# Spreading the rows of later blocks over eleven steps, and routing in seven groups instead of six

## The chip, the cores and the metric

The kernel is one program on one core of a Trainium2 chip. The metric is the device time of one launch in microseconds (us); less is better. The engines are named as the profile names them: PE is TensorE (PEld its weight loads), DVE VectorE, ACT ScalarE, POOL GpSimd, SP SyncE.

## What is computed

Pooled attention, then a sparse layer with 8 experts of which each row takes 2, then a dense layer with 4 experts that all rows take. There are N = 2304 rows of D = 512. Cut to what matters:

```python
x = attention(q, k, v)                       # 18 tiles of 128 rows
noisy = x @ w_gate + log1p(exp(x @ w_noise)) * noise
top2, weights = best two experts of each row, softmax of their noisy logits
for e in range(8):                           # first layer: each row by its two experts
    out[mask] += w * (relu(x[mask] @ w1[e]) @ w2[e])
p = domain_probs / sum(domain_probs)
for e in range(4):                           # second layer: all rows by all four experts
    out2 += p[:, e] * (relu(out @ w1b[e]) @ w2b[e])
```

## The kernel before

Everything is ordered by hand: each engine has its own list of instructions and waits on semaphores; nothing is scheduled for it. Products in float32 are made as three matmuls of a high part and a low part (`PASSES`), so each operand is needed twice: ACT makes the high part, DVE or POOL the low one.

**Attention and routing (0 to 150 us).** One turn of a loop for each of the 18 tiles. `GROUPS` says after which tiles the routing of a group is done: ACT `softplus(g)` one turn after its last tile, DVE `select(g)` two turns after, PE `ranks(g)`, DVE `places(g)` and `pair_weights(g)` three turns after. With the places known, POOL's `scatter(g)` issues two indirect DMAs for each tile into `x_sorted`. Only when all 36 have landed does ACT load the first sorted rows.

**First layer (150 to 660 us).** 44 tiles at most, of which the last ones may be empty; an empty tile is skipped by a branch on each engine (`guarded`). ACT stores each tile with `y_store`. Behind it POOL waits for all stores and then gathers.

**Second layer (660 us to the end).** The 2304 rows are three blocks of 768 (blocks 0, 1, 2), the weights 16 units (`UNITS`: 4 experts in 4 quarters), visited twice. Steps 0 to 15 (`SOLO`) are block 0 with units 0 to 15. Steps 16 to 47 are blocks 1 and 2 with each unit in turn (`double`). A step is one `up` (a Strassen-like product of 7 parts, 42 matmuls, with sums on DVE, `hidden`) and one `down` (36 matmuls in six outputs, `accumulate` on DVE). PE's order is up(s), down(s-1), up(s+1), down(s), and so on. The output banks are a ring of three, so output t waits until DVE has added output t-3.

Around the steps there are two other jobs:

- The operands of a block are made from nine pairs of rows tiles. `fetch(n)` on POOL gathers the two expert results of rows tile n (two indirect DMAs), `scale_first(n)` on ACT and `combine(n)` on DVE add them with their weights, `x2_turn(n)` on PE transposes them, and `pair_hi`, `sums_hi` (ACT), `pair_sums`, `pair_lo` (DVE) make the operands of pair i = tiles 2i and 2i+1. Pairs 0 to 2 are block 0, 3 to 5 block 1, 6 to 8 block 2. Block 1's operands are first read in step 16. Pair 6 and later overwrite those of block 0.
- The weights of unit n: SP loads them, POOL makes `weight_sums`, ACT `w1_high(n)` and `w2_high`, POOL `w1_low` and `w2_low`. `up` of the unit waits for `w1_ok`, `down` for `w2_ok`.

Before, pairs 3, 4 and 5 are made in steps 1 to 3, and rows tiles 12 to 16 in a bunch before steps 14 and 15. POOL starts the weight sums of unit n only when PE has finished the last `up` that reads the buffer (`pool.wait_ge(up_ps, used)`). In each step DVE first finishes the hidden block, with its last two low parts, and then adds the six outputs.

## Time and profile before

| | |
|---|---|
| three runs | 1496.77 us median (1495.77 to 1503.64) |
| the profiled execution | 1504.66 us, of which its span is 1502.6 us |
| PE busy | 1373.0 us (91%) |
| DVE busy | 717.5 us (48%) |
| POOL busy | 647.4 us (43%) |
| ACT busy | 398.0 us (26%) |
| chain that ended last | PE 45%, DVE 3%, issue 2%, POOL, ACT and DMA 1% each |

The profile is of one execution, so times inside it are compared with its own 1504.66 us, not with the median. Its page lists a slot as busy when a matmul is under way, whatever the clock; the granted clock is listed beside it.

### The profile page before, as it was taken

Reading aid. Unit: us, or ns where it says so; the run is one execution under the profiler, and the core shown is the slowest. Engines: PE = TensorE matmul, PEld = TensorE weight load, DVE = VectorE, ACT = ScalarE, POOL = GpSimd, SP = SyncE. Lnnn points to the kernel's source line nnn. Section 1 sums busy time; section 2 is a strip of 40 time slices with the busy share of each in tenths; the row PEclk is TensorE's granted clock in tenths of the full one; section 3 lists DMA queues with packets and bytes.
Section 4 is the critical chain, followed back from the end, with each engine's and each line's share of the span. In section 5 each row is a group of like instructions: output and inputs, shape, how many; then the busy total and the mean of one; then the engine's idle time right before and its main releaser. Section 6 shows DMA issues by size and latency. Waiting matters only on the chain.

```text
span 1502.6 us, 22621 instructions
## 1 busy us (share of the span) xinstructions
PE 1373.0 (91%) x6969; PEld 1206.9 (80%) x6970; DVE 717.5 (48%) x1287; ACT 398.0 (26%) x734; POOL 647.4 (43%) x421
## 2 busy tenths in 40 slices
PE   6884799999999999954589999889999999999999
PEld 5884688888888888844469999779898989989897
DVE  5657422222222222215466666676666565665655
ACT  2443122222222222213233333332222222222311
POOL 1226357275382662724446667633332234222320
PEclk9887799999999999976789999999999999999999
DMA  9737233242332422222212213220010000100002
GB/s 272 254 108 277 73 127 115 82 154 84 112 130 74 151 98 98 85 86 77 72 55 70 70 56 113 92 90 28 29 56 28 28 28 28 55 28 28 14 0 84
DMA packets 64105, 131.86 MB, mean 88 GB/s; under 512 B 4984, under 2 KB 22520, under 8 KB 63992
## 3 DMA queue, kind: packets, MB, share of 16 engines
q1 hardware_dynamic: 45432, 86.79, 17.1%
q0 software_dynamic: 6528, 22.42, 4.8%
q10 hardware_dynamic: 12096, 22.03, 4.3%
q8 instruction: 27, 0.44, 0.1%
q14 instruction: 22, 0.18, 0.0%
HBM read 106.57 MB, written 28.84 MB: 90 GB/s over the span
## 4 chain that ended last, share of the span: by engine, by line
PE 45%; DVE 3%; issue 2%; POOL 1%; ACT 1%; DMA 1%; DVEq 0%; POOLq 0%; ACTq 0%
PE banks L851 24%; PE banks L824 21%; DMA acc<-y_sorted,y_pos_int 1%; POOL unit_w_ops L487 1%; DVE hD L1580 1%; DVE acc L1618 0%; POOL acc L526 0%; DVE x_ops L1576 0%; DVE acc L1551 0%; DVE x_sums L1562 0%; ACT block_sums L1123 0%; ACT hD L1129 0%; DVE x_sums L1565 0%; DVE x_sums L1563 0%; ACT acc L1095 0%
## 5 line engine op out<-in xcount | busy, mean ns | idle before, releaser
L851 PE MATMUL banks<-unit_w,hD 128*128 128x512 f32 x1728 | 405.8, 392 | 7.9 <-DVE acc L1618 6.2
L824 PE MATMUL banks<-x_ops,unit_w_ops 128*128 128x384 f32 x2016 | 368.4, 340 | 37.8 <-ACT block_sums L1123 29.0
L824 PEld LDWEIGHTS banks<-x_ops,unit_w_ops 128*128 128x128 f32 x2016 | 359.5, 192 | 43.9 <-ACT block_sums L1123 30.3
L851 PEld LDWEIGHTS banks<-unit_w,hD 128*128 128x128 f32 x1728 | 322.5, 188 | 78.5 <-DVE acc L1618 10.1
L1618 DVE SCALAR_TENSOR_TENSOR acc<-banks,prob_norm,acc 128x512 f32<-128x512 f32 x270 | 199.0, 747 | 95.0 <-PE banks L851 91.7
L748 PE MATMUL banks<-expert_w,xT 128*128 (+1 forms) x960 | 234.1, 400 | 1.6 <-DVE xT L1405 1.6
L774 PE MATMUL banks<-expert_w,hT 128*128 (+1 forms) x960 | 226.0, 391 | 2.8 <-issue 2.8
L774 PEld LDWEIGHTS banks<-expert_w,hT 128*128 128x128 f32 x960 | 181.3, 189 | 40.7 <-issue 3.0
L748 PEld LDWEIGHTS banks<-expert_w,xT 128*128 128x128 f32 x960 | 180.7, 192 | 39.5 <-issue 1.9
L1518 DVE COPY y_rows<-banks 128x512 f32<-128x512 f32 x40 | 27.6, 691 | 338.9 <-PE banks L774 338.9
L544 POOL TENSOR_TENSOR expert_w<-raw_weights,zeros 128x2048 f32 x28 | 100.8, 3600 | 191.6 <-PE banks L774 173.6
L469 POOL TENSOR_TENSOR weight_sums<-raw_weights 128x256 f32<-128x256 f32 x32 | 24.1, 753 | 356.2 <-PE banks L824 308.7
L547 POOL TENSOR_TENSOR expert_w<-raw_weights,expert_w 128x2048 f32 x28 | 129.1, 4611 | 5.2 <-POOL expert_w L544 5.2
L1580 DVE SCALAR_TENSOR_TENSOR hD<-block_sums,hD 128x384 fp32r<-128x384 f32 x144 | 102.6, 739 | 34.3 <-ACT hD L1125 27.8
L1042 ACT CAST hT<-banks 128x512 fp32r<-128x512 f32 x80 | 43.0, 590 | 205.3 <-PE banks L757 205.3
L487 POOL TENSOR_TENSOR unit_w_ops<-raw_weights,unit_w_ops 128x512 fp32r<-128x512 f32 x64 | 63.7, 1017 | 65.2 <-ACT unit_w_ops L1139 65.1
L1033 ACT ACTIVATE h_rows<-banks 128x512 f32<-128x512 f32 x80 | 43.5, 596 | 181.0 <-PE banks L748 181.0
L491 POOL TENSOR_TENSOR unit_w<-raw_weights,unit_w 128x1024 fp32r<-128x1024 f32 x32 | 76.9, 2402 | 31.8 <-ACT unit_w L1144 31.6
L487 POOL TENSOR_TENSOR unit_w_ops<-weight_sums,unit_w_ops 128x1024 fp32r<-128x1024 f32 x32 | 76.8, 2400 | 0.0
L1507 DVE TENSOR_TENSOR hT<-banks,hT 128x512 fp32r<-128x512 f32 x80 | 51.5, 686 | 50.1 <-ACT hT L1042 50.1
L1123 ACT COPY block_sums<-banks 128x384 f32<-128x384 f32 x48 | 23.0, 480 | 176.2 <-PE banks L824 169.6
L1125 ACT ACTIVATE hD<-block_sums 128x384 fp32r<-128x384 f32 x48 | 25.3, 526 | 152.9 <-DVE block_sums L1597 152.9
(177 smaller groups left out, 1202.7 us busy)
## 6 DMA issues: line engine op xcount, KB each, us to landing
raw_weights<-in_w SPq DMA_DIRECT2D x32, 1024.0 KB
raw_weights<-in_w1b SPq DMA_DIRECT2D x32, 512.0 KB, 3.4
raw_weights<-in_w2b SPq DMA_DIRECT2D x32, 512.0 KB, 3.2
x_rows<-x_sorted ACTq DMA_DIRECT2D x44, 256.0 KB, 2.6
y_sorted<-y_rows ACTq DMA_DIRECT2D x40, 256.0 KB, 2.0
out<-acc SPq DMA_DIRECT2D x18, 256.0 KB, 2.0
qT<-in_q SPq DMA_DIRECT2D x3, 1152.0 KB, 16.5
kv_half<-in_k SPq DMA_DIRECT2D x5, 576.0 KB, 11.6
```

The costliest lines, as they stand in the source:

```text
L487: ins = pool.tensor_tensor(lo, src, hi.bitcast(F32), ALU.subtract)
L491: pool.tensor_tensor(w2o[:, par, 1, :], raw[:, par, 1024:2048], w2o[:, par, 0, :].bitcast(F32), ALU.subtract).then_inc(w2_ok, 1)
L544: pool.tensor_tensor(hi, src, zeros[:, 0:1].to_broadcast([P, 2048]), ALU.add).then_inc(split_no, 1)
L547: pool.tensor_tensor(lo, src, hi.bitcast(F32), ALU.subtract).then_inc(raw_used[r % 2], 1)
L748: mm = pe.matmul(bank[n][:, :], xT[:, u % 2, st, c, :], wall[:, bass.ds(slot, 1), 0, mv, FF * c + 512 * n:FF * c + 512 * n + 512], start=( ...
L774: mm = pe.matmul(bank[5 + u % 2][:, :], hT[:, u % 2, st, c, :], wall[:, bass.ds(slot, 1), 1, mv, D * c:D * c + D], start=(t == 0), stop=(t ...
L824: mm = pe.matmul(dst[:, 0:HALF], w1o[:, par, st, b, c, :], x2o[:, blk, a, mv, c, :], start=(first and t == 0), stop=(t == 5), skip_group_c ...
L851: mm = pe.matmul(bank[5 + t % 3][:, :], hD[:, buf, st, c, P * t:P * t + P], w2o[:, par, mv, D * c:D * c + D], start=(n == 0), stop=(n == 3 ...
L1033: r = act.activation(h_sb[:, 512 * n:512 * n + 512], bank[n][:, :], ACT.Relu)
L1507: d = dve.tensor_tensor(hT[:, u % 2, 1, 4 * n:4 * n + 4, :], bank[2 + n][:, :].rearrange("p (c r) -> p c r", c=4), hT[:, u % 2, 0, 4 * n:4 ...
L1580: dve.scalar_tensor_tensor(out=hD[:, buf, 1, m, at:at + HALF], in0=src, scalar=0.0, in1=hD[:, buf, 0, m, at:at + HALF].bitcast(F32), op0=A ...
L1618: dve.scalar_tensor_tensor(out=to, in0=bank[5 + t % 3][:, :], scalar=p, in1=to, op0=ALU.mult, op1=ALU.add).then_inc(acc_ok, 1)
```

## The change

`GROUPS` gets seven entries instead of six, so that the third group is three tiles and ends one turn earlier. The rest moves work in the second layer:

- DVE: `hidden(s)` takes the outputs of step s-1 with it. Output 0 is added before the last two low parts, outputs 1 to 5 behind them. Extra work (a combine, or a part of a pair) stands behind a given output of a given step; the tables say which. Pairs 3, 4, 5 now come in steps 2, 4, 7, rows tiles 6 to 16 in steps 1, 3, 5, 6, 9, 10, 11.
- POOL: the weight sums no longer wait for PE; ACT's `w1_high` waits in their place.
- POOL no longer looks in the table of tiles which stores to wait for; ACT signals for the empty tiles in a branch.
- The operands of a pair are made in smaller pieces with a signal each, and `up(0)` starts with the products that need only the plain parts.

```diff
-GROUPS = ((0, 4), (4, 8), (8, 12), (12, 15), (15, 17), (17, 18))
+GROUPS = ((0, 4), (4, 8), (8, 11), (11, 13), (13, 15), (15, 17), (17, 18))
...
-            tail = [load_code(pool, j) for j in range(SURE_TILES, TILES_B)]
-            pool.wait_ge(y_out[0], 16 * SURE_TILES // 2)
-            pool.wait_ge(y_out[1], 16 * SURE_TILES // 2)
-            for j in range(SURE_TILES, TILES_B):
-                with pool.If(tail[j - SURE_TILES] // 16 % 2 > 0):
-                    pool.wait_ge(y_out[j % 2], 16 * (j // 2 + 1))
+            for i in range(2):
+                pool.wait_ge(y_out[i], 16 * TILES_B // 2)
...
+            for n in range(2, SOLO + 2):
+                if n == 2:
+                    pool.wait_ge(x2T_ps, BT)
+                    for r in range(BT, BT + 3):
+                        fetch(r)
+                w1_sums(n, n % 2, n // 2 + 1)
...
+                w1_lows(n, n % 2)
+                if n == 3:
+                    pool.wait_ge(x2_ok, BT + 2)
+                    fetch(BT + 3)
...
+                if n > 2:
+                    w2_of(n - 1, (n - 1) % 2)
+                if n == 9:
+                    pool.wait_ge(x2T_ps, 2 * BT)
+                    for r in range(2 * BT, 2 * BT + 3):
+                        fetch(r)
...
-            up(0, 0, 0)
+            product(0, 0, A11, B11, bank[0]).then_inc(up_ps, 1)
+            product(0, 0, A22, T4, bank[4])
+            pe.wait_ge(m1_ok, 1)
+            product(0, 0, A12, B21, bank[0], first=False)
+            pe.wait_ge(x2_sum_hi, 6)
             pairs_read(3)
+            product(0, 0, S2, T2, bank[1]).then_inc(up_ps, 1)
+            product(0, 0, S3, T3, bank[2]).then_inc(up_ps, 1)
+            product(0, 0, S1, T1, bank[3]).then_inc(up_ps, 2)
+            pe.wait_ge(cx, 3)
+            product(0, 0, S4, B22, bank[3], first=False).then_inc(up_ps, 1)
+
+            turns = {2: 3, 4: 4, 7: 5}
+            for n in range(1, 8):
                 pe.wait_ge(w1_ok, n + 1)
-                pairs_read(n + 1 if n > 1 else 3)
+                if n - 1 in turns:
+                    pairs_read(turns[n - 1] + 1)
                 up(n, n % 2, 0)
-                pair_turn(n + 2)
+                if n in turns:
+                    pair_turn(turns[n])
                 pe.wait_ge(w2_ok, n)
                 down(n - 1, (n - 1) % 2, (n - 1) % 2)
...
+                with act.If(codes[u] // 16 % 2 > 0):
+                    y_store(g, u)
+                with act.Else():
+
+                    act.wait_ge(y_out[u % 2], 16 * (j // 2))
+                    act.sem_inc(y_out[u % 2], 16)
...
+            scaled = {1: (6, 7), 3: (8, 9), 5: (10,), 6: (11,), 9: (12, 13), 10: (14, 15), 11: (16,), 15: (17,)}
+            turned = {2: 3, 4: 4, 7: 5, 15: 6, 16: 8}
+            for s in range(SOLO):
+                h_hi_d(s, s % 2)
+                if s in turned:
+                    pair_hi(turned[s])
+                    sums_hi(turned[s])
+                for n in scaled.get(s, ()):
+                    scale_first(n)
+                w1_high(s + 2, s % 2, 6 * s + 6)
+                if s:
+                    w2_high((s + 1) % 2, (s + 1) // 2 + 1, BT * s)
...
+                if outputs:
+                    outputs(0)
                 dve.wait_ge(hD_hi, 4 * s + 3)
                 low(buf, 0, HALF, three)
                 dve.wait_ge(hD_hi, 4 * s + 4)
                 low(buf, 1, 0, both)
+                if outputs:
+                    for t in range(1, BT):
+                        outputs(t)
...
+            extras = {1: rows_in(6, 7), 2: pair_in(3), 3: rows_in(8, 9), 4: pair_in(4), 5: rows_in(10), 6: rows_in(11),
+                      7: pair_in(5), 9: rows_in(12, 13), 10: rows_in(14, 15), 11: rows_in(16)}
```

**How the order moves.** First ACT, from the end of the hidden block of step 0 to the start of that of step 1. In the rows `acc<-acc,pair_weights` is `scale_first`, `unit_w_ops` are the three casts of `w1_high(2)`, and `block_sums<-banks` is the copy in `h_hi_d(1)` on whose signal PE waits in `up(1)`. Before:

```order
L1129 ACTIVATE hD<-block_sums 128x384
L1131 ACTIVATE hD<-block_sums 128x384
L1095 ACTIVATE acc<-acc,pair_weights 128x512 x3
L1137 CAST unit_w_ops<-raw_weights 128x512
L1138 CAST unit_w_ops<-raw_weights 128x256
L1139 CAST unit_w_ops<-weight_sums 128x1024
L1095 ACTIVATE acc<-acc,pair_weights 128x512
L1123 COPY block_sums<-banks 128x384
```

And after the change:

```order
L1141 ACTIVATE hD<-block_sums 128x384
L1143 ACTIVATE hD<-block_sums 128x384
L1151 CAST unit_w_ops<-raw_weights 128x512
L1152 CAST unit_w_ops<-raw_weights 128x256
L1153 CAST unit_w_ops<-weight_sums 128x1024
L1135 COPY block_sums<-banks 128x384
```

The four `scale_first` (rows tiles 6 to 9) no longer stand ahead of the copy; the three casts still do.

Then DVE in step 1: `block_sums` and `hD` are the hidden block, `acc<-banks,prob_norm` an output of step 0, `acc<-acc,pair_weights` a `combine`, `x_sums` and `x_ops` a pair. Before:

```order
L1591 TENSOR_TENSOR block_sums<-banks,block_sums 128x384
L1594 TENSOR_TENSOR block_sums<-banks,block_sums 128x384
L1597 TENSOR_TENSOR block_sums<-banks,block_sums 128x384
L1580 SCALAR_TENSOR_TENSOR hD<-block_sums,hD 128x384
L1580 SCALAR_TENSOR_TENSOR hD<-banks,hD 128x384
L1603 TENSOR_TENSOR block_sums<-block_sums,banks 128x384
L1605 TENSOR_TENSOR block_sums<-block_sums,banks 128x384
L1580 SCALAR_TENSOR_TENSOR hD<-block_sums,hD 128x384 x2
L1551 SCALAR_TENSOR_TENSOR acc<-acc,pair_weights 128x512
L1562 TENSOR_TENSOR x_sums<-banks,x_sums 128x256
L1563 TENSOR_TENSOR x_sums<-banks,x_sums 128x256
```

And after the change:

```order
L1576 TENSOR_TENSOR block_sums<-banks,block_sums 128x384
L1559 SCALAR_TENSOR_TENSOR hD<-block_sums,hD 128x384
L1559 SCALAR_TENSOR_TENSOR hD<-banks,hD 128x384
L1582 TENSOR_TENSOR block_sums<-block_sums,banks 128x384
L1584 TENSOR_TENSOR block_sums<-block_sums,banks 128x384
L1605 TENSOR_SCALAR acc<-banks,prob_norm 128x512
L1559 SCALAR_TENSOR_TENSOR hD<-block_sums,hD 128x384 x2
L1605 TENSOR_SCALAR acc<-banks,prob_norm 128x512
L1523 SCALAR_TENSOR_TENSOR acc<-acc,pair_weights 128x512
L1605 TENSOR_SCALAR acc<-banks,prob_norm 128x512
L1523 SCALAR_TENSOR_TENSOR acc<-acc,pair_weights 128x512
L1605 TENSOR_SCALAR acc<-banks,prob_norm 128x512 x3
```

The pair has left the step, the first output stands ahead of the last two low parts, and the two combines stand between later outputs.

## Rows read from the trace of the kernel before

**Rows 1.** Windows: stretch, length, busy PE, PEld, DVE, ACT, POOL, PEclk, DMA share, GB/s

```profile
705.00:790.00 85.00, 55.99 (x259) 48.59 (x260) 45.63 (x73) 26.98 (x48) 39.69 (x35) 0.84 0.16 56
...
922.00:1010.00 88.00, 77.67 (x372) 67.18 (x372) 61.99 (x96) 31.96 (x56) 49.26 (x42) 0.96 0.28 93
...
1010.00:1503.00 493.00, 489.38 (x2455) 442.35 (x2453) 299.92 (x472) 117.73 (x212) 143.84 (x113) 1.00 0.10 34
```

**Rows 2.** Waits of TensorE: engine, line, releaser, total us, times, longest

```profile
PE banks L824 <- ACT block_sums L1123: 29.0, 4, 13.0
...
PE banks L729 <- DMA x_rows<-x_sorted: 17.5, 1, 17.5
```

**Rows 3.** Timeline, TensorE, first steps of the second layer (start, us, what, idle before)

```profile
704.99 4.40 PE L824 MATMUL banks<-x_ops,unit_w_ops 128*128 128x384 f32 x24 [1.26 <-DVE block_sums L1605]
...
722.38 6.13 PE L824 MATMUL banks<-x_ops,unit_w_ops 128*128 128x384 f32 x18 [12.98 <-ACT block_sums L1123]
...
771.73 7.47 PE L824 MATMUL banks<-x_ops,unit_w_ops 128*128 128x384 f32 x42
...
789.96 7.47 PE L824 MATMUL banks<-x_ops,unit_w_ops 128*128 128x384 f32 x42
```

**Rows 4.** The chain that ended last, one undisturbed step (start, us, what)

```profile
821.23 7.30 PE banks L824 x42
828.53 8.23 PE banks L851 x36
```

**Rows 5.** Timeline, ScalarE, just before TensorE's wait at 722 us ends

```profile
721.24 0.72 ACT L1095 ACTIVATE acc<-acc,pair_weights 128x512 f32<-128x512 f32 x1 [12.01 <-DMA acc<-y_sorted,y_pos_int]
```

**Rows 6.** Timeline, GpSimd, the weight sums of one unit: first and last

```profile
703.87 0.73 POOL L469 TENSOR_TENSOR weight_sums<-raw_weights 128x256 f32<-128x256 f32 x1 [6.08 <-issue]
...
706.38 0.93 POOL L474 TENSOR_TENSOR weight_sums<-weight_sums,raw_weights 128x256 f32<-128x256 f32 x1
```

**Rows 7.** Timeline, TensorE, the steps around the change of blocks

```profile
929.83 7.47 PE L824 MATMUL banks<-x_ops,unit_w_ops 128*128 128x384 f32 x42
...
989.36 4.43 PE L824 MATMUL banks<-x_ops,unit_w_ops 128*128 128x384 f32 x24
...
1009.84 7.47 PE L824 MATMUL banks<-x_ops,unit_w_ops 128*128 128x384 f32 x42
```

**Rows 8.** Timeline, GpSimd's scatters, and the first gather behind them

```profile
129.80 0.96 POOL L453 DMA_INDIRECT x_sorted<-x_sb,pos_int  x1 [1.66 <-DVE pos_int L1366]
...
146.05 1.14 POOL L453 DMA_INDIRECT x_sorted<-x_sb,pos_int  x1 [0.30 <-issue]
...
151.87 0.39 ACTq L1017 DMA_DIRECT2D x_rows<-x_sorted  x1
```

**Rows 9.** Timeline, last store and first fetch; from the page, a store's landing

```profile
661.16 0.36 ACTq L1049 DMA_DIRECT2D y_sorted<-y_rows  x1
...
665.36 0.99 POOL L526 DMA_INDIRECT acc<-y_sorted,y_pos_int  x1 [34.43 <-issue]
...
y_sorted<-y_rows ACTq DMA_DIRECT2D x40, 256.0 KB, 2.0
```

**Rows 10.** Timeline, block 0: last transpose, last low parts (DVE), first product

```profile
688.49 1.11 PE L810 MATMUL banks<-ident,acc 128*128 128x128 f32 x4 [1.61 <-DVE acc L1551]
...
693.25 1.22 DVE L1576 TENSOR_TENSOR x_ops<-x_sums,x_ops 128x1024 fp32r<-128x1024 f32 x1 [0.18 <-ACT x_ops L1113]
...
694.74 8.99 PE L824 MATMUL banks<-x_ops,unit_w_ops 128*128 128x384 f32 x42 [5.14 <-DVE x_ops L1576]
```

**Rows 11.** Timeline, VectorE's low part of a hidden block, alone and beside GpSimd

```profile
857.76 0.56 DVE L1580 SCALAR_TENSOR_TENSOR hD<-block_sums,hD 128x384 fp32r<-128x384 f32 x1 [0.59 <-ACT hD L1125]
...
935.23 2.41 POOL L491 TENSOR_TENSOR unit_w<-raw_weights,unit_w 128x1024 fp32r<-128x1024 f32 x1
...
935.45 2.60 DVE L1580 SCALAR_TENSOR_TENSOR hD<-block_sums,hD 128x384 fp32r<-128x384 f32 x1 [0.59 <-ACT hD L1125]
```

**Rows 12.** Timeline, ScalarE, a late start in the attention stage

```profile
99.71 0.79 ACT L935 COPY expT<-banks 96x768 f32<-96x768 f32 x1 [5.50 <-remote]
```

254 lines of the change are left out of this document (86 added, 168 removed).

## The prediction

> **What bounds the kernel now.** I read the windows first. From 1010 us to the end PE is busy without a gap at full clock; it is not in the 85 us from 705, where the clock is 0.84 and PE is busy for 56.0, nor in the 88 us from 922, where it is busy for 77.7 [rows 1]. The chain of waits confirms that full stretches are PE's own time: one undisturbed step is 7.30 us of `up` and 8.23 us of `down`, 15.53 in all, with nobody else in it [rows 4]. So only what refills PE in the disturbed stretches can give time.
>
> The waits by releaser name two large ones: 29.0 us in four waits for the copy of the block sums on ACT, and 17.5 us in one wait for the first sorted rows [rows 2]. The timeline shows the longest of the four: 24 matmuls of `up(1)` from 704.99, then 12.98 us of nothing, then 18 matmuls that take 6.13 us [rows 3]. At the full clock 18 of 42 are 18/42 x 7.30 = 3.13 us, so the wait also costs 3.0 us of clock. The copy is short, but on ACT it stands behind a `scale_first` that began only at 721.24, after 12.01 us in which ACT had nothing to do but wait for its rows to land [rows 5]. The bound there is the order on ACT, not its load.
>
> **The change, term by term** (against the profiled execution's 1504.66 us).
>
> *Routing, -2.7.* Before, twelve scatters run from 129.80 to 146.05, the last start: (146.05 - 129.80)/11 = 1.48 us each, and the gather of rows is issued 151.87 - 146.05 = 5.8 us behind the last start [rows 8]. These twelve are tiles 12 to 17. With the new groups tile 12 goes with (11, 13), whose places come two turns earlier, in time that POOL has free; ten scatters stay behind the places of (13, 15), which come in the same turn as before. That is two scatters less: 2 x 1.48 = 3.0. The seventh group costs DVE, PE and ACT some small instructions in the turns before, so I take -2.7; its bounds are -1.4 (one scatter) and -4.5 (three). Behind it stands the 17.5 us wait, so it shortens one to one.
>
> *End of the first layer, +2.* The last store is issued at 661.16 and lands 2.0 us later; the first fetch is issued at 665.36 [rows 9]. Of the 2.2 us between, some 0.3 is the start, as between two scatters, so POOL's last branch in and its four for the empty tiles take 1.9, about 0.4 each. They go, but ACT must now walk through its own before it gives the last signal: behind the store 12 guarded pieces and two loads of the table. No row times one of these; at POOL's 0.4 each, 661.52 + 14 x 0.4 = 667.1, and the fetch 0.3 behind, 2 us later than now. Lower bound: they hide behind the landing, and POOL's saved branches give 1 us. Upper bound: ACT's are half as dear again, +5. I take +2, by the nearest row.
>
> Advanced Engine Details and Errata of the Trainium skill (Control Flow Timing) gives about 108 ns for a compare-and-branch and 51 ns for a jump; by that the term would be about zero. No row here shows it.
>
> *Operands of block 0 and up(0), -2.6.* The last transpose starts at 688.49, the first product at 694.74, right behind the low parts of the sums; these start at 693.25 for 1.22 us, after DVE had stood 0.18 [rows 10]. The plain low parts were ready at 693.07. The new order starts with products that need only these: 694.74 - 693.07 = 1.7 less. The signals are finer too: the first sum starts a transpose early, and casts and low parts of the sums overlap by halves. I put that at about 0.6 in each of the three rounds, an estimate from pieces of 0.3 to 0.6 us (bounds 0 and 1): 1.7 + 1.7 = 3.4. Inside `up(0)` the last product now waits for a DVE sum (0.56 for such a size [rows 11], and the way there and back) that the two plain products used to cover: +0.8.
>
> *First refill, -30.* From the start of `up(1)`, 704.99, to that of `up(4)`, 789.96, are 84.97 us [rows 3] for three steps. The step with pair 5, 771.73 to 789.96, is 18.23 [rows 3], so a pair costs 18.23 - 15.53 = 2.7: eight transposes and the outputs that DVE adds late. New: three steps and one pair, 3 x 15.53 + 2.7 = 49.3. Two pairs are paid later: + 5.4. 84.97 - 49.3 - 5.4 = 30.3.
>
> This needs that nothing new is late at `up(1)`. ACT: the hidden block of step 0, then the three casts of `w1_high(2)` (about 2 us), then the copy. PE runs 24 matmuls, 4.40 us, before it needs the copy, and 1.26 us pass before it starts [rows 3]. ACT ends the hidden block about 2 us behind `up(0)` (four short pieces, DVE sums of 0.56 between them): 2 + 2 + 0.5 = 4.5 against 5.66. POOL: the weight sums that the casts wait for take 706.38 + 0.93 - 703.87 = 3.4 us [rows 6] behind six fetches of about 1.3 us, together 11.3 from the last transpose, while `up(0)` alone ends some 12.5 from there. No wait, with 1.2 us to spare on each side. Rows tiles 6 and 7 have one step more to land, tile 9 two.
>
> *Change of blocks, -10.5.* From 929.83 to 1009.84 [rows 7] are 80.0 us for four ups and four downs. New: 4 x 15.53 = 62.1, two pairs 5.4, two more transposes 0.8, and about 1.2 for the last product of `up(16)` behind the sums: 69.5. The rows are combined in steps 9 to 11; a late tile can't hold the copy, and output 0 is added before the low parts, so a held-up low part no longer holds PE. `up(16)` keeps its place, 989.36, relative to pair 6: pair 7 can't be made before the banks of the outputs are free.
>
> *A pair in its new place, +1.* The low parts of a pair now stand behind output 2, not 0, and the next `up` waits for them: by my count of DVE's work they end 8.5 us into a `down` of 8.2 to 9. Five pairs, 0.2 each; bounds 0 and +5.
>
> *Everything else, 0.* The weight sums start earlier in each step, beside other work of DVE; PE needs the weights a step later. Output 0 lands about 2.2 us into a `down`, and the ring needs it at 4.1.
>
> Sum: -2.7 + 2 - 2.6 - 30.3 - 10.5 + 1 = -43. On the profiled execution 1504.66 - 43 = 1461.6. That execution was 7.9 above the median; the trace doesn't show where, and I take none of it as removed. So on the median 1496.77 - 43 = **1454**.
>
> **Rivals.**
>
> *A wait takes the place of the first (12 in 100).* The margins at `up(1)` are about 1 us. If the fetches are slow, ACT stands before the weight sums instead of before the rows, and PE's clock falls again. The waits at the change of blocks still go. The worst likely is one wait of half the old size with its clock, 12.98/2 + 3 = 9.5, and as much in a later step: about -43 + 19 = -24, **1473**. For it: POOL's queue is serial, and ACT's too. Against: nothing lands late in the count above.
>
> *Instruction supply (8 in 100).* The loops of ACT, DVE and POOL over steps 4 to 13 become straight code. ACT starts a copy at 99.71 after 5.50 us idle that no wait explains [rows 12], in straight code while the DMA queues are full. Two such gaps, with little hidden by slack, add 4 to 8: **1458 to 1462**. Runtime: NRT & Kernel Launch of the Trainium skill (Instruction fetch mechanics) says that straight code is fetched ahead and a taken branch out of the window is what stalls; by that rule this change gains at the loops and the new branches of ACT lose. The trace shows only the gap, not its cause.
>
> *Slower (4 in 100): DVE and POOL hold each other in every step.* A low part of the hidden block takes 0.56 us alone and 2.60 while POOL's subtraction runs [rows 11]. The weight sums now start beside this low part, in 46 steps. Followed through the step, output 0 would be ready at about 2.9 instead of 2.2 us; the ring asks for it at 4.1, so a hold of 2.04 costs nothing. It costs from about 2.9 us of hold on, and to eat 43 us and end **above 1504** it must be 2.9 + 50/46 = 4.0 us in each step. Two of POOL's 2.41 us instructions in a row would do it. GPSIMD Engine Reference of the Trainium skill (1. Specifications) says that the two share SBUF interfaces when a DVE instruction has two SBUF inputs, as this one has; the row agrees, and the rule speaks against moving the sums.
>
> *No effect (4 in 100).* The stretches are as long as before, because the rows, not ACT's order, set them: **1490 to 1500**. Against: ACT waits for rows of block 1, which no product reads before step 16.
>
> **How the numbers follow.** Forecast 72 in 100, its own range 1446 to 1463 from the bounds: routing +1.3 and -1.8, stores -3 and +3, pairs -1 and +4, change of blocks +3 and -2. The range to state reaches to the first rival, 1445 to 1470. About 0.5% (7.5 us) is what a measurement of this kernel tells from no change. Faster 0.92, same 0.04, slower 0.04.
>
> **What would show it.** Right: no wait over 2 us for the copy of the block sums, full clock from the second product of the layer on, steps of 15.5 us with 18 in steps 2, 4 and 7; the first gather about 149; the first fetch 6 us behind the last store. Wrong: ACT waiting for weight sums or rows inside steps 1 to 3, low parts of a pair ahead of an `up` that waits, low parts of 3 us and more in each step beside POOL, or idle without a releaser in the straight code.

## The result and the profile after

The changed kernel takes 1458.05 us (median of 4 runs, 1455.32 to 1460.38); the kernel before took 1496.27 us beside it (4 runs). The ratio is 0.974, with a 95% interval of 0.9694 to 0.9785: faster. The forecast was 1454 us, range 1445 to 1470.

The profiled execution of the changed kernel took 1460.38 us (its span is 1458.7 us), which is 44.3 us less than the 1504.66 us of the profiled execution before. The forecast by terms, made for that pair, was -43, or 1461.6 us. The medians differ by 38.2 us only; the interval of the ratio allows 32 to 46 us, and the experiments show what scatters (below).

The page of the changed kernel, its busy PE and the granted clock in 40 slices:

```profile
PE 1361.3 (93%) x6970; PEld 1197.4 (82%) x6971; DVE 706.5 (48%) x1310; ACT 396.8 (27%) x746; POOL 638.0 (44%) x421
PE   6885699999999999992999999999999999999999
PEclk9977799999999999995999999999999999999999
```

One weak slice is left at the border of the two layers. The timeline of TensorE there, for the changed kernel (start us, us, what, and in brackets the idle time before and who ended it):

```profile
690.03 8.57 PE L818 MATMUL banks<-x_ops,unit_w_ops 128*128 128x384 f32 x36 [2.89 <-issue]
699.25 1.32 PE L818 MATMUL banks<-x_ops,unit_w_ops 128*128 128x384 f32 x6 [0.65 <-DVE block_sums L1576]
701.84 7.54 PE L818 MATMUL banks<-x_ops,unit_w_ops 128*128 128x384 f32 x42 [1.26 <-DVE block_sums L1584]
...
717.42 7.47 PE L818 MATMUL banks<-x_ops,unit_w_ops 128*128 128x384 f32 x42
724.73 1.04 PE L804 MATMUL banks<-ident,acc 128*128 128x128 f32 x8
725.52 8.75 PE L845 MATMUL banks<-unit_w,hD 128*128 128x512 f32 x36
735.14 7.55 PE L818 MATMUL banks<-x_ops,unit_w_ops 128*128 128x384 f32 x42 [0.88 <-issue]
...
750.73 7.47 PE L818 MATMUL banks<-x_ops,unit_w_ops 128*128 128x384 f32 x42
```

Against [rows 3]: the wait inside `up(1)` and the slow 18 matmuls behind it are gone, and from the start of `up(1)` to that of `up(4)` are 750.73 - 701.84 = 48.89 us, not 84.97. The one pair in these three steps, turned at 724.73, costs a `down` of 8.75 us and 0.88 us of wait ahead of the next `up`.

The windows of the changed kernel, the first steps of the second layer and the long last stretch (columns as in [rows 1]):

```profile
701.84:787.00 85.16, 83.40 (x424) 74.57 (x424) 61.86 (x99) 36.52 (x65) 60.02 (x49) 1.00 0.23 78
965.30:1458.70 493.40, 489.33 (x2455) 442.46 (x2454) 289.10 (x474) 116.15 (x212) 133.28 (x109) 1.00 0.10 35
```

In the same length in which PE was busy for 56.0 us at a clock of 0.84 [rows 1] it is busy for 83.4 at full clock.

At the change of blocks the kernel before lost the most in `up(15)`, again by a row that ScalarE scales ahead of the copy. These are its TensorE and its ScalarE there:

```profile
972.54 5.79 PE L824 MATMUL banks<-x_ops,unit_w_ops 128*128 128x384 f32 x18 [3.88 <-ACT block_sums L1123]
```

```profile
970.46 0.72 ACT L1095 ACTIVATE acc<-acc,pair_weights 128x512 f32<-128x512 f32 x1 [9.73 <-DMA acc<-y_sorted,y_pos_int]
```

In the changed kernel nothing waits for the copy there. Inside `up(16)` a wait of 2.25 us is left, and the timeline shows where it is from, first on TensorE, then on VectorE:

```profile
944.40 6.50 PE L818 MATMUL banks<-x_ops,unit_w_ops 128*128 128x384 f32 x36
953.15 1.62 PE L818 MATMUL banks<-x_ops,unit_w_ops 128*128 128x384 f32 x6 [2.25 <-DVE block_sums L1576]
```

```profile
947.95 2.21 DVE L1552 TENSOR_TENSOR x_ops<-x_sums,x_ops 128x512 fp32r<-128x512 f32 x1
950.08 1.22 DVE L1555 TENSOR_TENSOR x_ops<-x_sums,x_ops 128x512 fp32r<-128x512 f32 x1
951.22 0.55 DVE L1570 TENSOR_TENSOR block_sums<-banks,block_sums 128x384 f32<-128x384 f32 x1
951.87 0.56 DVE L1573 TENSOR_TENSOR block_sums<-banks,block_sums 128x384 f32<-128x384 f32 x1
952.53 0.56 DVE L1576 TENSOR_TENSOR block_sums<-banks,block_sums 128x384 f32<-128x384 f32 x1
```

Pair 7's low parts (L1552, L1555) take 2.21 and 1.22 us there beside GpSimd, where pair 6's took 0.68 each, and three block sums stand behind them; the last product of `up(16)` needs the third of these.

Last, the end of the first layer in the changed kernel, the last store on ScalarE's queue and the first fetch on GpSimd:

```profile
658.46 0.35 ACTq L1057 DMA_DIRECT2D y_sorted<-y_rows  x1
```

```profile
663.99 0.99 POOL L526 DMA_INDIRECT acc<-y_sorted,y_pos_int  x1 [35.64 <-ACTq L1084]
```

5.53 us lie between them, against 4.20 in [rows 9]; GpSimd is released by L1084, the signal in ScalarE's `Else`.

### The profile page after: what moved, and what is told of

The parts are those of the page before. It is cut to its first block, busy times and chain, and to the rows that moved or that the text cites. A ratio compares the mean times of both kernels' runs of the same rounds, so it can differ in the third digit from the quotient of the medians.

```text
span 1458.7 us, 22255 instructions
## 1 busy us (share of the span) xinstructions
PE 1361.3 (93%) x6970; PEld 1197.4 (82%) x6971; DVE 706.5 (48%) x1310; ACT 396.8 (27%) x746; POOL 638.0 (44%) x421
## 4 chain that ended last, share of the span: by engine, by line
PE 51%; DVE 2%; issue 1%; DMA 0%; ACT 0%; POOL 0%; DVEq 0%; POOLq 0%
PE banks L845 26%; PE banks L818 24%; PE banks L804 1%; DVE acc L1602 0%; DVE x_ops L1555 0%; DVE acc L1523 0%; DMA acc<-y_sorted,y_pos_int 0%; POOL acc L526 0%; DVE hD L1559 0%; DVE x_ops L1552 0%; DVE x_sums L1536 0%; DVE x_ops L1544 0%; DVE x_ops L1546 0%; ACT x_ops L1118 0%; DVE x_sums L1538 0%
## 5 line engine op out<-in xcount | busy, mean ns | idle before, releaser
L818 PE MATMUL banks<-x_ops,unit_w_ops 128*128 128x384 f32 x2016 | 361.8, 337 | 10.0 <-issue 4.7
L818 PEld LDWEIGHTS banks<-x_ops,unit_w_ops 128*128 128x128 f32 x2016 | 353.6, 189 | 15.9 <-issue 9.0
L487 POOL TENSOR_TENSOR unit_w_ops<-raw_weights,unit_w_ops 128x512 fp32r<-128x512 f32 x64 | 67.7, 1078 | 363.8 <-ACT unit_w_ops L1153 363.7
L1559 DVE SCALAR_TENSOR_TENSOR hD<-block_sums,hD 128x384 fp32r<-128x384 f32 x144 | 87.7, 637 | 28.6 <-ACT hD L1137 28.4
L453 POOL DMA_INDIRECT x_sorted<-x_sb,pos_int x36 | 37.1, 1031 | 55.6 <-DVE pos_int L1338 46.2
```

The lines of the kernel that those rows point to most:

```text
L487: ins = pool.tensor_tensor(lo, src, hi.bitcast(F32), ALU.subtract)
L818: mm = pe.matmul(dst[:, 0:HALF], w1o[:, par, st, b, c, :], x2o[:, blk, a, mv, c, :], start=(first and t == 0), stop=(t == 5), skip_group_c ...
L1559: dve.scalar_tensor_tensor(out=hD[:, buf, 1, m, at:at + HALF], in0=src, scalar=0.0, in1=hD[:, buf, 0, m, at:at + HALF].bitcast(F32), op0=A ...
```

## A ruler for the experiments

The whole times were taken in three groups, by the record on three chips: b_again, before_order, sums_wait and out0_last on chip 4; before_orders, bunched2, pool_asks and six_groups on chip 6; banks_only, up0_old, best1 and best2 on chip 14. The kernel before took 1497.02, 1487.96 and 1497.16 us beside them. So whole times compare across groups only as ratios to the kernel before, and the absolute times that some expectations name are some 9 us too high for the second group.

Single terms are smaller than what whole runs scatter, so each is read between two landmarks inside the trace. They are: the last product of the routing's gate on TensorE; the first gather; the last store of the first layer; the first fetch; the starts of `up(0)`, `up(1)`, `up(8)`, `up(15)`, `up(17)`; the end. In us, from the starts of the rows (the first five columns are lengths):

| kernel | gate to gather | store to fetch | fetch to up(1) | up(1) to up(8) | up(17) to end | gate at | gate to end |
|---|---|---|---|---|---|---|---|
| before | 20.28 | 4.20 | 39.63 | 147.14 | 492.8 | 131.59 | 1371.0 |
| before, again | 20.34 | 4.19 | 39.81 | 146.73 | 492.8 | 131.50 | 1368.1 |
| changed | 18.42 | 5.53 | 37.85 | 115.77 | 493.4 | 131.87 | 1326.8 |
| before_order | 20.08 | 4.20 | 41.28 | 138.19 | 492.9 | 126.01 | 1363.7 |
| before_orders | 20.88 | 4.20 | 39.71 | 122.11 | 492.5 | 110.92 | 1346.2 |
| sums_wait | 18.57 | 5.53 | 38.76 | 117.36 | 493.4 | 129.84 | 1332.7 |
| out0_last | 18.40 | 5.54 | 37.96 | 113.49 | 492.2 | 131.63 | 1322.9 |
| bunched2 | 18.79 | 5.54 | 37.86 | 117.03 | 493.4 | 119.74 | 1326.6 |
| pool_asks | 18.48 | 4.19 | 38.50 | 117.35 | 493.4 | 113.49 | 1327.9 |
| six_groups | 20.92 | 5.56 | 37.97 | 115.77 | 493.4 | 114.72 | 1329.5 |
| banks_only | 18.67 | 5.54 | 38.63 | 113.75 | 493.4 | 139.88 | 1327.2 |
| up0_old | 18.50 | 5.54 | 37.41 | 115.76 | 494.5 | 128.44 | 1327.4 |
| best1 | 18.59 | 4.18 | 38.57 | 112.77 | 492.2 | 135.95 | 1320.0 |
| best2 | 13.81 | 4.18 | 37.16 | 111.21 | 492.3 | 134.07 | 1312.5 |

The column "gate at" is the stage that no experiment touches but for its groups, and it spreads over 29 us: 110.92 to 119.74 us on chip 6, 126.01 to 139.88 us in all others. "Gate to end" leaves it out. Where `up(1)` itself takes 9.1 us in place of 7.5 (sums_wait, pool_asks, banks_only, best1), the clock is at its full level later; below this is called the late clock. The windows from 701 to 709 us of the changed kernel and of sums_wait, both around `up(1)`:

```profile
701.00:709.00 8.00, 7.16 (x41) 7.19 (x42) 4.97 (x9) 4.15 (x8) 4.72 (x4) 1.00 0.00 0
```

```profile
701.00:709.00 8.00, 6.93 (x31) 6.96 (x32) 4.34 (x8) 3.53 (x7) 5.94 (x7) 0.79 0.00 0
```

Nearly the same busy time holds 41 matmuls at a clock of 1.00 and 31 at 0.79. That is worth some 2.2 us over `up(0)` and `up(1)` (pool_asks against the changed kernel). No edit is common to the four kernels that have it, and pool_asks changes nothing there; what decides it was not tested.

## The experiments

### The kernel before, once more

> The kernel before, unchanged, profiled once more: to see which stretches vary from one execution to the next. Its profiled execution took 1504.66 us where the median of its runs is about 1496. If the surplus of 8 us sat in the first refill, the second trace shows less than 84.97 us from the start of up(1) to that of up(4), and the forecast gain there was too large by as much. If it sat in the routing stage (TensorE's waits for ScalarE's transposes and VectorE's keys), the refill is again 84 to 86 us and the stretch up to the first gather (151.87 us) is shorter by some microseconds. If the long last stage held it, the 492.76 us from up(17) to the end shrink.

It took 1501.71 us. The refill is as long as in the first trace: from `up(1)`, 702.22, to `up(4)`, 786.81, are 84.59 us. The gate stands at 131.50. The 3.0 us that this execution is shorter lie in the first layer, between the first gather and the last store. So the two executions differ outside the part that the change touches. Where the other 5 of the 8 us over the median lie is open, since this execution is above its median too.

### Only row 9, only on ScalarE (in the kernel before)

```diff
             w1_high(2, 0)
-            scale_first(BT + 3)
             h_hi_d(1, 1)
+            scale_first(BT + 3)
             pair_copy(3)
```

> The kernel before with one line moved: ScalarE scales row 9 behind its four copies of the hidden values of step 1 and no longer ahead of them. Theory (ScalarE's order held the copies behind a row that had not landed): the wait of 12.98 us inside up(1) [rows 3] is gone, and with it part of the low clock behind it: 10 to 16 us faster than before, about 1481 to 1486 us; the waits for rows 10 and 11 stay or shrink. Rival one (GpSimd's weight sums, which waited for the products of the step before, set the pace of the refill): no more than 3 us gained, the wait moves to the weights. Rival two (rows simply land too late for whoever needs them): the time of the wait comes back at the turn of pair 4, less than 5 us gained.

1489.5 us where before took 1497.02, ratio 0.9939 (0.9915 to 0.9964): 7.5 us in the median, and 8.5 us between `up(1)` and `up(4)`, 76.09 where the second trace of before has 84.59. That is less than the 10 to 16 expected of the theory and more than either rival gave. The timeline of TensorE in this kernel says why:

```profile
705.50 3.41 PE L824 MATMUL banks<-x_ops,unit_w_ops 128*128 128x384 f32 x18 [0.23 <-ACT block_sums L1123]
...
720.61 7.00 PE L851 MATMUL banks<-unit_w,hD 128*128 128x512 f32 x18 [6.74 <-DVE acc L1621]
...
742.68 5.17 PE L824 MATMUL banks<-x_ops,unit_w_ops 128*128 128x384 f32 x18 [10.88 <-ACT block_sums L1123]
```

and of its ScalarE and VectorE:

```profile
716.51 0.72 ACT L1095 ACTIVATE acc<-acc,pair_weights 128x512 f32<-128x512 f32 x1 [4.66 <-DMA acc<-y_sorted,y_pos_int]
717.14 0.35 ACT L1102 COPY x_sums<-banks 128x256 f32<-128x256 f32 x1
...
741.54 0.72 ACT L1095 ACTIVATE acc<-acc,pair_weights 128x512 f32<-128x512 f32 x1 [7.63 <-DMA acc<-y_sorted,y_pos_int]
```

```profile
717.35 0.75 DVE L1551 SCALAR_TENSOR_TENSOR acc<-acc,pair_weights 128x512 f32<-128x512 f32 x1 [3.77 <-ACT acc L1095]
```

The 12.98 us wait is 0.23 now. But VectorE also works in order: it combines row 9 at 717.35, makes the sums of pair 3 and adds the outputs of `down(0)` only behind that, so `down(0)` stands 6.74 us for a free bank. Those sums need copies of the pair as well, and on ScalarE these still stand behind row 9 (717.14). So the row holds VectorE twice, by its own combine and by ScalarE's copies of the pair; no run parts the two. And `up(2)` still waits for the copy that stands behind row 11. Half of the first stall came back one product later.

### Three rows on ScalarE, two of them on VectorE (in the kernel before)

```diff
@@ ScalarE
-            scale_first(BT + 3)
             h_hi_d(1, 1)
             ...
             w1_high(3, 1)
-            scale_first(BT + 4)
+            scale_first(BT + 3)
             w2_high(0, 2, BT)
-            scale_first(BT + 5)
             h_hi_d(2, 0)
+            scale_first(BT + 4)
             ...
             w1_high(4, 0)
+            scale_first(BT + 5)
@@ VectorE
             hidden(1, 1)
-            combine(BT + 3)
             pair_in(3, 0, 0)
-            combine(BT + 4)
+            combine(BT + 3)
             hidden(2, 0)
+            combine(BT + 4)
             pair_in(4, 1, 1)
```

(Row 11 keeps its place on VectorE, behind pair 4.)

> The kernel before with rows 9, 10 and 11 taken in later on both engines that work in order: ScalarE scales row 9 behind the hidden copies of step 1 and the pair turned there, row 10 behind the copies of step 2, row 11 behind that step's pair; VectorE combines each of them behind the outputs that stood behind it. GpSimd's late weight sums, the steps in which pairs are turned and everything else stay as before. From the kernel with row 9 moved on ScalarE alone, which went from up(1) to up(4) in 76.1 us (84.6 in the kernel before again) with a wait of 6.74 us for VectorE behind row 9 and one of 10.88 us behind row 11. Theory (the place of the rows in the order of both engines is the cause): both are gone and up(1) to up(4) takes 53 to 60 us, the whole 1468 to 1476 us. Rival (a row needs three pairs in three steps too soon, so that the changed kernel's spread over eight steps is what pays): the waits come back at the turns of pairs 4 and 5, up(1) to up(4) takes 68 us or more, the whole over 1482 us.

1462.68 us where before took 1487.96 beside it, ratio 0.9843 (0.981 to 0.9875). From `up(1)` to `up(4)` are 684.12 to 744.05, 59.9 us, at the upper end of the theory's 53 to 60; up to `up(8)` it is 122.11 us. In medians it is 25 us faster than before, so order alone brings 25 of the changed kernel's 31 us there (147.14 - 122.11 of 147.14 - 115.77). No wait of over 2.3 us is left in the first steps:

```profile
699.00 1.66 PE L851 MATMUL banks<-unit_w,hD 128*128 128x512 f32 x6 [1.84 <-DVE acc L1621]
701.72 3.02 PE L851 MATMUL banks<-unit_w,hD 128*128 128x512 f32 x12 [1.06 <-DVE acc L1621]
...
721.50 4.49 PE L851 MATMUL banks<-unit_w,hD 128*128 128x512 f32 x12 [2.24 <-DVE acc L1618]
```

These are outputs 1 and 2 of a `down`, late behind the pair's sums on VectorE, since output 0 and the pair stand there in one block. The changed kernel puts each part of a pair behind an output of its own, which fits the other 6 us; no run isolates it.

### GpSimd's weight sums wait again (in the changed kernel)

```diff
-            def w1_sums(n, par, turn):
+            def w1_sums(n, par, turn, used):
                 pool.wait_ge(w1_in[par], 16 * turn)
+                pool.wait_ge(up_ps, used)
```

> The changed kernel with GpSimd's weight sums of a step waiting again until the products of the step two before have been taken in, as in the kernel before. Theory (the order on ScalarE was the cause, the earlier sums are worth little): 0 to 3 us slower than the changed kernel, that is 1458 to 1461 us, the loss at the first one or two steps, where the weights come about 3.4 us behind up(0). Rival (the earlier sums are what freed the refill): 13 us or more slower, and TensorE waits for the weights' last operands at every step from up(1) on.

1462.76 us, ratio 0.9762 (0.972 to 0.9803), just above the theory's 1458 to 1461. From `up(2)` to `up(8)` it takes 819.43 - 719.20 = 100.2 us, in the changed kernel 817.61 - 717.42 = 100.2: nothing. `up(1)` is 1.6 us longer, by its clock (above), and from `up(15)` to `up(17)` 2.0 us are lost, 41.05 against 39.03. The rival's 13 us are not there. The earlier sums are worth about 2 us, at the change of blocks.

### Output 0 last (in the changed kernel)

```diff
                 dve.tensor_tensor(both, both, bank[3][:, 0:HALF], ALU.add).then_inc(cx, 1)
-                if outputs:
-                    outputs(0)
                 ...
                 low(buf, 1, 0, both)
                 if outputs:
-                    for t in range(1, BT):
+                    for t in range(BT):
                         outputs(t)
```

> The changed kernel with VectorE adding output 0 to the accumulator behind the last two low parts of the hidden values again, not ahead of them. Theory: in the long last stage nothing waits for that output, so the 493 us of it stay within 1 us; in the steps that turn a pair TensorE's products of down wait less or as long for the hidden values (the low parts come 0.56 us earlier) and the pair's sums start later by as much: within 2 us of the changed kernel, 1456 to 1460 us. Rival (the place of output 0 is what let the pairs go in without a wait): 5 us or more slower, with waits for the pair's operands ahead of up(3), up(5) and up(8).

1458.4 us, ratio 0.9743 (0.9718 to 0.9768): the same in whole runs. In the traces the new place of output 0 costs a little. A step that turns a pair, first in the changed kernel, then with output 0 last:

```profile
807.63 8.77 PE L845 MATMUL banks<-unit_w,hD 128*128 128x512 f32 x36
817.61 7.57 PE L818 MATMUL banks<-x_ops,unit_w_ops 128*128 128x384 f32 x42 [1.21 <-DVE x_ops L1555]
```

```profile
806.31 8.46 PE L845 MATMUL banks<-unit_w,hD 128*128 128x512 f32 x36
815.29 7.54 PE L818 MATMUL banks<-x_ops,unit_w_ops 128*128 128x384 f32 x42 [0.52 <-DVE x_ops L1555]
```

`down` is 0.31 us shorter and the wait for the pair's low parts 0.69. From `up(1)` to `up(8)` that makes 2.3 us. From `up(8)` to `up(13)` 1.0 us is lost (78.60 against 77.64), at the change of blocks 1.7 are gained (68.39 against 70.05 from `up(13)` to `up(17)`), in the last stretch 1.2 (492.2 against 493.4); gate to end is 3.9 us less. It was expected within 2 us; the sign is against the changed kernel.

### The pairs closer together (in the changed kernel)

```diff
-            turns = {2: 3, 4: 4, 7: 5}
+            turns = {2: 3, 3: 4, 5: 5}
-            extras = {1: rows_in(6, 7), 2: pair_in(3), 3: rows_in(8, 9), 4: pair_in(4), 5: rows_in(10), 6: rows_in(11),
-                      7: pair_in(5), 9: rows_in(12, 13), 10: rows_in(14, 15), 11: rows_in(16)}
+            extras = {1: rows_in(6, 7), 2: {**pair_in(3), 3: lambda: combine(8), 4: lambda: combine(9)},
+                      3: {**pair_in(4), 3: lambda: combine(10)}, 4: rows_in(11), 5: pair_in(5), 9: rows_in(12, 13), 10: rows_in(14, 15), 11: rows_in(16)}
```

(ScalarE's `scaled` and `turned` and GpSimd's fetches go along.)

> The changed kernel with the pairs of the first refill turned at steps 2, 3 and 5 and not at 2, 4 and 7, and rows 8 and 9 taken in at step 2, 10 at step 3 and 11 at step 4, with their fetches as much earlier. Theory (a row's place behind the copies in the order of ScalarE and VectorE counts, the spread does not): the whole refill from up(1) to up(8) stays within 4 us of the changed kernel's 115.8 us, total 1456 to 1462 us. Rival (the spread itself is needed, rows land too late for closer steps): waits of 5 us or more ahead of the turns of pairs 4 or 5, total over 1464 us.

Ratio 0.9736 (0.9698 to 0.9775), the same as the changed kernel's 0.974. From `up(1)` to `up(8)` are 117.03 us, 1.3 more, and as much is gained from `up(13)` to `up(17)`, 68.5 against 70.1. No wait in these steps is longer than 1.1 us, where the rival had 5 or more. The spread over eight steps is not what pays.

### GpSimd asks again (in the changed kernel)

```diff
-            for i in range(2):
-                pool.wait_ge(y_out[i], 16 * TILES_B // 2)
+            tail = [load_code(pool, j) for j in range(SURE_TILES, TILES_B)]
+            pool.wait_ge(y_out[0], 16 * SURE_TILES // 2)
+            pool.wait_ge(y_out[1], 16 * SURE_TILES // 2)
+            for j in range(SURE_TILES, TILES_B):
+                with pool.If(tail[j - SURE_TILES] // 16 % 2 > 0):
+                    pool.wait_ge(y_out[j % 2], 16 * (j // 2 + 1))
@@ ScalarE, behind the guarded store
-                with act.Else():
-                    act.wait_ge(y_out[u % 2], 16 * (j // 2))
-                    act.sem_inc(y_out[u % 2], 16)
```

> The changed kernel with GpSimd's branches over the tiles that may be empty put back, and ScalarE's Else taken out. In the changed kernel the time from the issue of the first layer's last store to the first fetch of a row is 5.53 us, in the kernel before 4.20 us. Theory (ScalarE's walk through the Else branches before the last wait is passed costs what GpSimd's branches cost and more): back to 4.2 us, 1.3 us less than the changed kernel and 0 to 1 us in the total beyond what scatters from run to run. Rival (the difference is in how long the last store's landing takes, or chance): still 5.2 us or more.

From last store to first fetch it takes 4.19 us:

```profile
640.31 0.36 ACTq L1061 DMA_DIRECT2D y_sorted<-y_rows  x1
```

```profile
644.50 0.99 POOL L526 DMA_INDIRECT acc<-y_sorted,y_pos_int  x1 [34.36 <-issue]
```

So the `Else` costs 1.34 us more than the branches on GpSimd. The ratio is 0.9689 (0.9655 to 0.9724), which looks like some 7 us against the changed kernel's 0.974. But the intervals overlap, and by the trace no more than 1.3 us are this edit's: gate to end is 1327.9, 1.1 us more than in the changed kernel (by the late clock), and the gate stood at 113.49.

### Six groups (in the changed kernel)

```diff
-GROUPS = ((0, 4), (4, 8), (8, 11), (11, 13), (13, 15), (15, 17), (17, 18))
+GROUPS = ((0, 4), (4, 8), (8, 12), (12, 15), (15, 17), (17, 18))
```

> The changed kernel with the routing in six groups of 4, 4, 4, 3, 2 and 1 tiles again. The first turn of the first layer stood at 154.56 us in the kernel before and at 153.00 us in the changed one (152.85 with output 0 placed last). Theory (the groups let the scatters of tiles 8 to 14 start earlier): the first turn is at 154.2 to 155.5 us, the total 1 to 3 us above the changed kernel. Rival (scatters wait on something else, or attention's own waits moved the start): first turn within 0.5 us of 153.0 us.

The first turn was at 138.29 us, neither in the theory's window nor in the rival's, since the gate came at 114.72 and not at 131.87; the absolute landmark was badly chosen. From the gate it is clear. TensorE, GpSimd and ScalarE's queue with six groups:

```profile
114.72 1.89 PE L667 MATMUL banks<-gate_w,x_sbT 128*128 128x16 f32 x8 [0.86 <-ACT x_sbT L961]
```

```profile
130.46 0.97 POOL L453 DMA_INDIRECT x_sorted<-x_sb,pos_int  x1 [0.30 <-issue]
```

```profile
135.64 0.39 ACTq L1025 DMA_DIRECT2D x_rows<-x_sorted  x1
```

and with seven, in the changed kernel:

```profile
131.87 1.89 PE L667 MATMUL banks<-gate_w,x_sbT 128*128 128x16 f32 x8 [1.29 <-ACT x_sbT L961]
```

```profile
142.53 2.31 POOL L453 DMA_INDIRECT x_sorted<-x_sb,pos_int  x1 [0.30 <-issue]
```

```profile
150.29 0.39 ACTq L1025 DMA_DIRECT2D x_rows<-x_sorted  x1
```

Gate to gather is 20.92 and 18.42 us. Over all traces but best2, five with six groups give 20.08 to 20.92, mean 20.50, and eight with seven give 18.40 to 18.79, mean 18.55: the groups bring 1.95 us. The ratio, 0.9724 (0.9689 to 0.9759), doesn't show them against the changed kernel's 0.974.

### Up(0) as it was (in the changed kernel)

```diff
-            product(0, 0, A11, B11, bank[0]).then_inc(up_ps, 1)
-            product(0, 0, A22, T4, bank[4])
-            pe.wait_ge(m1_ok, 1)
-            product(0, 0, A12, B21, bank[0], first=False)
             pe.wait_ge(x2_sum_hi, 6)
             pairs_read(3)
-            ...
+            up(0, 0, 0)
```

> The changed kernel with up(0) as it was: all products behind the last pair's low parts, in the old order. In the changed kernel up(0) starts 26.0 us behind the first fetch and lasts 11.8 us to the start of up(1); before it started 29.4 us behind the first fetch and lasted 10.3 us. Theory (two products brought ahead of the last low parts): up(0) starts 28 to 29.4 us behind the first fetch, up(1) 38.0 to 39.5 us behind it where it was 37.85, so 0.2 to 1.7 us are lost. Rival (the split of the pair's sums alone brought the gain): up(1) stands at 37.8 us or less behind the first fetch.

```profile
687.75 8.98 PE L818 MATMUL banks<-x_ops,unit_w_ops 128*128 128x384 f32 x42 [4.14 <-DVE x_ops L1547]
697.83 7.52 PE L818 MATMUL banks<-x_ops,unit_w_ops 128*128 128x384 f32 x42 [1.10 <-DVE block_sums L1576]
```

It took 1457.45 us in one run. `up(0)` starts 27.33 us behind the fetch (660.42), `up(1)` 37.41. The theory fell: the new `up(0)` starts 1.3 us earlier (26.04) and loses 1.7 up to the start of `up(1)`, so `up(1)` is 0.4 us later with it. What was gained at this place against before, 39.63 to 37.41, is left for the finer signals and halves; no run takes these out.

Where the 1.7 us go can be read. The windows from the start of `up(0)` for as long as its matmuls come at the lower clock, in the changed kernel and in up0_old:

```profile
690.03:694.33 4.30, 4.30 (x14) 4.30 (x15) 1.09 (x2) 0.48 (x1) 3.38 (x4) 0.50 0.65 174
```

```profile
687.75:690.76 3.01, 3.01 (x9) 3.01 (x10) 0.00 (x0) 0.48 (x1) 2.10 (x4) 0.50 0.63 180
```

TensorE does not stop there in either; but with the new order it runs 4.30 us at half the clock and not 3.01, so of the earlier start some 0.65 us are spent at half speed. The last product then waits 0.65 us for the block sum, and the rest, some 0.4 us, is the start behind that wait and a wait ahead of `up(1)` of 1.26 and not 1.10. The clock's part varies: with the same new order `up(0)` to `up(1)` takes 11.03 us in best2, 11.81 in the changed kernel and 12.56 in banks_only, so the 0.4 us is a comparison of two executions and no more.

### Waiting only for the banks (in the changed kernel)

```diff
+            def banks_read(i):
+                pe.wait_ge(x2_hi, 2 * i)
+                pe.wait_ge(x2_plain, i)
@@ in up, behind the first product
+                if turned is not None:
+                    banks_read(turned)
@@ in the steps behind pairs 3 to 7, in place of
-                    pairs_read(turns[n - 1] + 1)
```

> The changed kernel with one alteration: TensorE waits, between two steps, only until the two turned banks have been read and no longer for the low parts of the pair's sums. Theory: the waits of 0.88 us ahead of up(3) and up(5) and of 1.21 us ahead of up(8) are gone, up(1) to up(8) falls from 115.8 to 112.8 to 113.5 us. Rival (the step is bound by VectorE's whole work, so the time is given back inside the next up): up(1) to up(8) stays within 1 us of 115.8 us, with waits for block sums inside up.

It took 1468.79 us in one run, with the gate at 139.88. From `up(1)` to `up(8)` are 113.75 us, `up(1)` at the late clock among them; from `up(2)` on it is 825.86 - 729.24 = 96.6 against 100.2. The waits ahead of `up(3)`, `up(5)` and `up(8)` are gone, and nothing was given back: from `up(8)` to `up(13)` it takes 77.64 us, as in the changed kernel.

### Four edits together

best1 is banks_only with output 0 last, GpSimd's branches, and pair 7's low parts behind the block sums of step 16:

```diff
+                if ahead:
+                    ahead()
                 dve.wait_ge(hD_hi, 4 * s + 3)
                 low(buf, 0, HALF, three)
@@
-            pair_lo(7)
-            hidden(SOLO, 0, accumulate(SOLO - 1, 0, (SOLO - 1) // QUARTERS, 1, pair_in(8)))
+            hidden(SOLO, 0, accumulate(SOLO - 1, 0, (SOLO - 1) // QUARTERS, 1, pair_in(8)), lambda: pair_lo(7))
```

> The changed kernel with four places altered: GpSimd's branches in place of ScalarE's Else (1.34 us less from last store to first fetch, measured alone), output 0 behind the last low parts again (2.3 us less from up(1) to up(8), measured alone), TensorE waits ahead of the next up only for the reads of the two turned banks and no longer for the low parts of the pair's sums (0.5 to 0.9 us at each of the pairs 3, 4, 5), and the low parts of pair 7's sums are made behind the third and fourth block sums of step 16 and not ahead of the first (wait inside up(16) 2.25 us, 3.23 us with output 0 last). Theory: up(1) to up(8) 112 us, up(15) to up(17) 34 to 35.5 us where it was 39.0, no wait for block sums inside up(16), ratio to before 0.966 to 0.971. Rival (the low parts then come late for up(17), or VectorE's work ahead of the hidden values holds down(16)): up(16) to up(17) stays above 19 us and the ratio stays at 0.972 or more.

1450.02 us, ratio 0.9676 (0.9648 to 0.9704). The wait inside `up(16)` is gone:

```profile
946.25 7.72 PE L826 MATMUL banks<-x_ops,unit_w_ops 128*128 128x384 f32 x42
```

`up(15)` to `up(17)` is 963.76 - 929.05 = 34.71 us, 39.03 in the changed kernel. `up(1)` to `up(8)` is 112.77 with the late clock. But from `up(8)` to `up(13)` 2.1 us are given back, 79.77 against 77.64: in the steps where rows tiles 12 to 15 are combined, TensorE waits up to 1.42 us for VectorE's outputs, which now start behind the low parts. Gate to end is 6.8 us less than in the changed kernel.

### And the last quarter of the first expert's weights later

```diff
             dve.tensor_tensor(tab[:, 0, :], t44[:, 5, :], t44[:, 2, :], ALU.mult).then_inc(rows_ok, 1)
-            for half in range(2):
-                low_half(3, half)
             ...
+            for half in range(2):
+                low_half(3, half)
             x_lo(0, 0)
```

> The kernel with four places altered, and a fifth: VectorE makes the low parts of the last quarter of the first expert's weights (two operations of 1.2 us) not while GpSimd still issues the last scatters but in its idle 7.6 us behind them. In the changed kernel the scatter beside those operations took 2.31 us where others take 0.97, and it was the last. Theory: the last scatter takes 0.97 to 1.1 us and the time from the last product of the gate to the first gather, 18.4 to 18.8 us in kernels with seven groups, falls by 1.3 us. Rival (the low parts then come late for the first products, or what lands last is not the last scatter): the first product of the first layer stands as far behind the last gate product as before, no gain.

1449.65 us, ratio 0.9662 (0.9618 to 0.9706), the fastest here by its ratio; its interval overlaps that of best1, and the medians are only 0.4 us apart. In the traces it is clearer. Gate to gather fell by 4.8 us (18.59 to 13.81), not by 1.3. GpSimd's last scatter, SyncE's queue and ScalarE's queue in best2:

```profile
144.73 1.02 POOL L453 DMA_INDIRECT x_sorted<-x_sb,pos_int  x1 [0.30 <-issue]
```

```profile
149.81 0.38 SPq L290 DMA_DIRECT2D raw_weights<-in_w  x1
```

```profile
147.88 0.39 ACTq L1037 DMA_DIRECT2D x_rows<-x_sorted  x1
```

In the changed kernel SyncE issues its load there at 144.16, because the low parts that read the buffer are done at 143.99, and the last scatter ends at 144.84:

```profile
144.16 0.38 SPq L290 DMA_DIRECT2D raw_weights<-in_w  x1
```

That load is of 1 MB, and until it has landed, 5.1 us later, the last scatter's rows have not landed either: the gather is released at 150.29, 5.45 us behind the scatter's end. In best2 the load goes out behind the gather, and the gather is released 147.88 - 145.75 = 2.13 us behind the end. So the later low parts gave 1.3 us by the shorter scatter and 3.3 us by an earlier landing. In each of the thirteen other traces such a load was issued before the last scatter ended, and the gather is released 4.0 to 5.8 us behind that end. It is not the slow issue that holds the landing: in six_groups the last scatter took 0.97 us, ends at 131.43, and its gather is released 4.21 us later; the load there was issued at 126.76 and takes 5 to 6 us. That the load is the cause is argued from this; no run moved the load alone. The first layer itself is as long as before (first turn to last store 505.6 us, 505.5 in the changed kernel), so all of it is kept up to there.

## Why the prediction was right, term by term

Measured between landmarks, changed minus before, with the terms in the prediction's order:

| term | forecast | in the pair of traces | what settled it |
|---|---|---|---|
| routing | -2.7 | -1.9 | six_groups: -1.95 over all traces |
| end of the first layer | +2 | +1.33 | pool_asks: 1.34 |
| operands of block 0 and up(0) | -2.6 | -1.8 | up0_old: -2.2 for the pieces, +0.4 for the new order |
| first refill, up(1) to up(8) | -30.3 | -31.4 | before_orders, bunched2 |
| change of blocks | -10.5 | -10.0 | sums_wait: 2.0 of it; no run takes the rest apart |
| a pair in its new place | +1 | in the two above | banks_only: the waits behind a pair cost 1.2 a pair |
| everything else | 0 | +0.6 behind up(17), +0.3 ahead of the gate, -1.1 from gather to last store, -0.1 from up(8) to up(13) | out0_last for the first: 1.2 of output 0; the others are scatter |
| sum | -43 | -43.9 of span | |

That the sum came within 1 us is in part luck. Routing and the operands were sized 0.8 us each too high, the end of the first layer 0.7 too dear, and the refill, the change of blocks and the pairs together brought 1.5 us more than forecast; most of these errors cancel.

**The main term** was right in mechanism and size. The long wait came from a late row that stood in a queue ahead of a copy. But the prediction put it down to "the order on ACT, not its load", and that was only the first half: before_order shows that with the copy of the block sums freed on ScalarE, VectorE holds the next product by the same row (6.74 us), and that row 11 holds ScalarE's copy one step on (10.88 us). With the rows moved on both engines, order alone gives 25 of 31 us. By sums_wait the late start of the sums on GpSimd is not part of it.

**The change of blocks** came as forecast in size. In the kernel before, `up(15)` waited 3.88 us for the copy behind a late row, and its last 18 matmuls then took 5.79 us, where 18/42 of 7.30 are 3.13; in the changed kernel that wait is gone. This is read from the two traces; that the rows' new place did it was not tested here by itself. The prediction gave 1.2 us to the last product of `up(16)`; it waits 2.25, behind pair 7's low parts. best1 shows that 4.3 us more were to be had there by VectorE's order.

**A pair in its new place.** Waits for a pair's low parts ahead of an `up`, a sign of being wrong by the prediction, are there: 0.88, 0.88 and 1.21 us, not 0.2 each. The steps with a pair are still shorter than the forecast 18.4 us, 17.7, 17.7 and 18.1, since TensorE no longer waits in `down` for outputs (1.28 us in the step with pair 5 before). So the time was right, and the wait in it was under-sized.

**Routing** was over-sized by 0.8 us. Two scatters went, 3.0 us by the count, but the places of group (13, 15) and the last scatter met VectorE's low parts of the weights and the 1 MB load behind them; the last start moved to 10.66 us behind the gate (142.53 - 131.87), from 14.46, so issue gained 3.8 us, and landing took back 1.9: 7.76 us from last start to gather, where it was 5.82 [rows 8]. The prediction had taken that last piece as fixed.

**The end of the first layer** was sized at GpSimd's 0.4 us a branch, the nearest row, and came to +1.33 instead of +2. By Advanced Engine Details and Errata of the Trainium skill (Control Flow Timing) the term was about zero; the 1.34 us of pool_asks don't bear that out, though ScalarE's path holds waits and semaphore updates beside its branches.

**up(0)**: the 1.7 us of an earlier start were right in kind (1.3), the loss inside was 1.7 instead of 0.8. The wait for the block sum, which the two plain products covered before, is as the prediction had it (0.65 us and the start behind it). What it left out is the clock: TensorE was at half its clock when `up(0)` began, and the earlier start bought matmuls at half speed, 14 of them in place of 9. So the step "starts with products that need only these: 1.7 less" gained nothing that these two executions show (+0.4). The 2.2 us that this place did gain are left for the finer signals.

**The rivals.** No wait took the place of the first, and `up(1)` ran without one; the margins of 1.2 us held. Instruction supply: in the straight steps 4 to 13 TensorE shows no gap over 1.3 us. Hold between VectorE and GpSimd: in the long last stretch the low part of the hidden values takes 576 ns in the mean (93 of them from 970 to 1450 us), where it took 688 before and takes 661 in sums_wait, so the earlier sums met it less, not more. Such holds stand elsewhere: pair 7's low part of 2.21 us, and the scatter of 2.31 us (0.97 alone). They cost where the held operation was the last in line. This agrees with the GPSIMD Engine Reference of the Trainium skill (1. Specifications), by which the two engines share SBUF interfaces.

**The median** was forecast 4 us too low: 1454 against 1458.05. The sum of -43 held for the two profiled executions. They stood 8.4 and 2.3 us above the medians of their kernels (1496.27, 1458.05). The forecast took the trace's gain over to the median as it was; this difference of 6 us, less the 1.3 us by which the trace's gain was larger than -43 and 0.5 us in the median before, is the miss. The kernel before scatters from 1480.44 to 1505.32 us over all its runs here. For all kernels together the table shows one place where such times lie, gate at 110.92 to 139.88 us, and it goes with the group: on chip 6, where the kernel before is 9 us faster, it is short in all four traces. From 60 to 110 us the granted clock is 0.96 to 1.00 in these four and 0.78 to 0.93 in the ten others. Whether it is the chip or the time of the group isn't shown. The windows from 60 us to the last gate, in before_orders and in the changed kernel, show both waits and clock in it:

```profile
60.00:110.92 50.92, 45.79 (x408) 44.04 (x406) 44.00 (x143) 32.30 (x67) 26.92 (x25) 0.99 0.58 214
```

```profile
60.00:131.87 71.87, 56.41 (x415) 53.88 (x413) 47.46 (x164) 33.81 (x71) 26.87 (x27) 0.83 0.51 188
```

The same work in 50.9 us at a clock of 0.99 and in 71.9 us at 0.83. In the longer one TensorE waits three times for 2.5 to 4.8 us for ScalarE, whose own wait ahead of one of them has no releaser on the core (5.04 us ahead of 95.25). As in [rows 12] the cause stays open.

## What to carry to other kernels

When an engine works in order and one of its instructions waits for a transfer that may be late, look on every engine that handles the same row, not only on the one named in the longest wait: here the row moved behind one copy on one engine brought 8.5 us, moved on both it brought 25. Place the late row behind everything that the busiest engine needs soon; how far it is spread over later steps mattered 1.3 us.

Read small terms between two landmarks on either side of the edit, never from the whole or from an absolute time. The stage ahead spread by 29 us, while gate to gather stayed within 0.8 us for the kernels with six groups and 0.4 for those with seven (best2 apart), so a term of 2 us could be read. And compare whole times only with the kernel before on the same chip.

An engine that starts earlier behind an idle stretch may only start at half its clock; price an earlier start at that speed.

A buffer that comes free starts a transfer. If small transfers that the critical path waits for are just landing, try to free a large load that is needed much later behind them, even by delaying the work that frees it; best2 gained 4.8 us from gate to gather by such a delay.

## What was unexpected of the hardware

- With a 1 MB load issued 0.7 us ahead of the end of the last scatter it took 5.45 us from that end to the release of the gather, and 2.13 us with the load behind the gather. That the load is the cause is likely, not shown.
- A scatter's issue on GpSimd takes 0.97 us, and 2.31 us beside VectorE's two low parts of 1.2 us.
- A routing stage of the same code took 110.92 to 139.88 us up to its last gate product, from one kernel to the next, and 110.92 to 119.74 on one of three chips.
- `up(0)`, started 1.3 us earlier behind the same kind of idle stretch, ran 4.30 us at half the clock in place of 3.01 us.
- ScalarE's `Else` path for four tiles that may be empty, at the end of the layer, took 1.34 us longer than GpSimd's branches over the same.
